# Expert operands of a fused attention and mixture-of-experts kernel, turned by VectorE's 32x32 blocks and by DMAs in place of TensorE

## The chip, the cores and the metric

The kernel runs on one core of a Trainium2 chip. The metric is the device time of one execution in microseconds, and lower is better. Before the change it is 1012.5 us, the median of three runs between 1011.4 and 1016.2.

## The reference

Three stages follow one another, all in float32. The attention lets a query see only the keys of its own bucket:

```python
mask = q_bucket[:, :, :, None] == k_bucket[:, :, None, :]
scores = np.where(mask, scale * np.matmul(q, k.transpose(0, 1, 3, 2)), -1000000000.0)
attn = softmax(scores)                     # batch 2, 8 heads, 768 tokens, head size 64
x = np.matmul(attn, v)                     # laid out as 1536 tokens x 512
```

The expert stage sends each of the 1536 tokens to the best two of 8 experts:

```python
noisy = x @ w_gate + np.log1p(np.exp(x @ w_noise)) * noise
for e in range(8):
    for k in range(2):
        mask = top2[:, k] == e
        h = np.maximum(x[mask] @ w1[e], 0.0)             # 512 -> 1024
        out[mask] += top2_w[mask, k, None] * (h @ w2[e])   # 1024 -> 512
```

The last stage computes `g(x @ w_in) @ w_out` for all tokens, with 2048 columns between and g a quotient of polynomials.

## The kernel before

The whole kernel is one block with a program for each engine, and semaphores between them; the order of work on an engine is the order in which its code is written. The change lies in the expert stage, between attention (to about 320 us) and the last stage (from about 715 us).

**Slots.** Tokens of one expert are gathered in tiles of 128 rows. There are 31 slots of one tile each, in the order of the experts; a table says which expert a slot has. With these inputs the experts 0 to 6 have 4, 3, 4, 3, 4, 4 and 3 slots, and expert 7 has the rest. `slots` unrolls the first and last slots and loops over the others, two at a time.

**One slot.** ScalarE issues the load of the tile's rows, `xg` (L766). TensorE turns them with 4 matmuls on the identity (`turn_x`, L1031) into `ps_m`. VectorE rounds the turned rows to a high part (L1405) and takes the remainder (L1407), both into `xT`. The up product (`up`, L1049) is 24 matmuls, three for each pair of 128 inputs and 512 outputs: high by high, high by remainder of the weights, remainder by high. It fills two banks, `ps_s0`. ScalarE applies relu into `h_sb` (L774), TensorE turns it by 8 matmuls (`turn_h`, L1060) into `ps_s1`, ScalarE rounds (L770) and VectorE takes the remainder (L1411) into `hT`. The down product (`down`, L1074) is 24 matmuls into one bank, `ps_o`; VectorE copies it to `y_sb` (L1417) and ScalarE stores it (L778). On TensorE slot i is: turn h of slot i-1, up product of i, turn x of i+1, down product of i-1.

**Weights.** `w_r` holds two experts in turn, each as a high part and a remainder. A fill (`fill`) belongs to GpSimd: it waits until the last up product of the expert before the previous one is done, issues two casting DMAs of 1 MB for the first half (L529), and splits the first two chunks: a split (L521) subtracts the high part from the raw chunk of 128x1024 and so needs both. Then it waits for that expert's last down product, issues the casts of the second half, and splits the other six chunks. The raw chunks go through a ring of two buffers; SyncE loads them (`stream`, L417), each as soon as the split of the chunk two before is done. After the slots the same code fills `w_out`; its first four splits stand in GpSimd's order behind the gathers of y (L630).

## Time and profile before

| | |
|---|---|
| median of three runs | 1012.5 us |
| profiled execution | 1014.4 us, of which the span is 1012.8 us |
| TensorE busy | 948.4 us, 94% of the span |
| VectorE, ScalarE, GpSimd busy | 593.4, 482.4, 402.4 us |
| moved by DMA | 134.4 MB, 133 GB/s in the mean |

The profile is of one execution. Busy time of an engine is an average over the stages; the chain of waits tells which engine's work sets the end in each of them. A landing is the time from the issue of a DMA until its data is there. The granted clock of TensorE is given as a share of 2.4 GHz.

### The profile page before, as it was taken

The page shows a single profiled execution, that of the slowest core. Times are in us where ns is not written, and L with a number is a line of the kernel's source. Part 1 is how long each engine was busy: PE and PEld are TensorE (multiplying, and loading weights), DVE is VectorE, ACT ScalarE, POOL GpSimd, SP SyncE. Part 2 cuts the span into 40 slices and gives each one's busy share as a digit, 9 for nine tenths or more (in the row PEclk, how much of TensorE's full clock was granted, in tenths as well). Part 3 has the DMA queues.
Part 4 walks back from the last instruction along what each step waited for, and adds up shares of the span by engine and source line. Part 5 has one row for each costly group of instructions (what it writes and reads, how often), then busy time and mean ns, then how long its engine had stood idle before and what let it go on. Part 6 is the DMA issues. An engine that isn't in the chain of part 4 may idle for free.

```text
span 1012.8 us, 17972 instructions
## 1 busy us (share of the span) xinstructions
PE 948.4 (94%) x5797; PEld 815.1 (80%) x5798; DVE 593.4 (59%) x1257; ACT 482.4 (48%) x883; POOL 402.4 (40%) x344
## 2 busy tenths in 40 slices
PE   6999999999891999999999999998489999999998
PEld 4888888888771788888888888887379999999997
DVE  7888888888766222222222222222289878878775
ACT  3677777777660111111111111111177777777775
POOL 4411120111244635544662636610477654463222
PEclk9999999999995999999999999999699999999999
DMA  9752324231133856857775748733621110100000
GB/s 200 220 162 69 84 47 98 52 84 54 63 126 134 282 181 233 286 180 260 266 254 182 248 166 277 282 105 115 194 68 62 33 62 21 53 25 17 32 1 31
DMA packets 102082, 134.42 MB, mean 133 GB/s; under 512 B 55698, under 2 KB 57746, under 8 KB 101522
## 3 DMA queue, kind: packets, MB, share of 16 engines
q1 hardware_dynamic: 73778, 63.01, 20.7%
q0 software_dynamic: 19328, 54.53, 16.4%
q10 hardware_dynamic: 8928, 16.26, 4.7%
q8 instruction: 28, 0.46, 0.2%
q14 instruction: 20, 0.16, 0.1%
HBM read 114.12 MB, written 19.66 MB: 132 GB/s over the span
## 4 chain that ended last, share of the span: by engine, by line
PE 82%; DVE 9%; issue 3%; ACT 2%; POOL 2%; DMA 2%; SPq 0%; DVEq 0%; another core or an unknown queue 0%; ACTq 0%; POOLq 0%
PE ps_s L1049 17%; PE ps_o L1074 17%; PE ps_s L1121 13%; PE ps_t L1107 6%; PE ps_t L919 4%; PE ps_o L932 4%; PE ps_s L1107 3%; PE ps_m L1107 3%; PE ps_s L1060 3%; PE ps_s L910 3%; DVE mx L1201 2%; PE ps_s L911 2%; PE ps_m L885 1%; PE ps_m L1031 1%; PE ps_o L944 1%
## 5 line engine op out<-in xcount | busy, mean ns | idle before, releaser
L521 POOL TENSOR_TENSOR w_r<-raw,w_r 128x1024 f32 (+1 forms) x72 | 171.6, 2399 | 95.9 <-DMA raw<-in_moe_w 41.1
L1049 PE MATMUL ps_s<-w_r,xT 128*128 x744 | 179.1, 397 | 1.8 <-DVE xT L1407 1.8
L1074 PE MATMUL ps_o<-w_r,hT 128*128 x744 | 177.3, 394 | 3.0 <-DVE hT L1411 2.6
L1049 PEld LDWEIGHTS ps_s<-w_r,xT 128*128 128x128 f32 x744 | 139.0, 190 | 29.8 <-issue 2.3
L1074 PEld LDWEIGHTS ps_o<-w_r,hT 128*128 128x128 f32 x744 | 137.5, 188 | 31.0 <-issue 3.5
L1121 PE MATMUL ps_s<-w_r,g_r 128*128 128x512 f32 x576 | 145.4, 397 | 4.5 <-DVE g_r L1491 4.5
L1121 PEld LDWEIGHTS ps_s<-w_r,g_r 128*128 128x128 f32 x576 | 107.6, 190 | 25.1 <-issue 4.3
L770 ACT ACTIVATE hT<-ps_s 128x1024 fp32r<-128x1024 f32 x31 | 31.8, 1027 | 174.3 <-PE ps_s L1060 87.8
L641 POOL TENSOR_TENSOR m<-q,g_r 128x384 f32<-128x384 f32 x64 | 65.9, 1030 | 113.6 <-DVE g_r L1479 113.3
L700 ACT ACTIVATE prob<-ps_s,nb,sc 128x768 f32<-128x768 f32 x96 | 95.3, 993 | 22.5 <-DVE nb L1206 21.8
L774 ACT ACTIVATE h_sb<-ps_s 128x1024 f32<-128x1024 f32 x31 | 31.8, 1027 | 151.8 <-PE ps_s L1049 151.8
L1417 DVE COPY y_sb<-ps_o 128x512 f32<-128x512 f32 x31 | 21.4, 691 | 137.2 <-PE ps_o L1074 137.2
L556 POOL TENSOR_TENSOR qm<-qs,nought 64x384 fp32r<-64x384 f32 x32 | 26.0, 819 | 175.5 <-DVE qs L1176 175.5
L1201 DVE TENSOR_REDUCE mx<-ps_s 128x1 f32<-128x768 f32 x96 | 91.4, 952 | 2.7 <-PE ps_s L911 1.0
L1405 DVE CAST xT<-ps_m 128x512 fp32r<-128x512 f32 x31 | 21.4, 692 | 118.5 <-PE ps_m L1031 118.5
L693 ACT ACTIVATE probT<-ps_t 128x768 f32<-128x768 f32 x93 | 74.9, 806 | 29.3 <-PE ps_t L919 29.3
L919 PE MATMUL ps_t<-ident,prob 128*128 128x128 f32 x570 | 79.6, 276 | 0.3 <-DVE probT L1233 0.3
L910 PE MATMUL ps_s<-km,qm 128*128 128x512 f32 x192 | 73.7, 385 | 0.1
L1107 PE MATMUL ps_t<-x2T,w_r 128*128 (+1 forms) x384 | 72.3, 337 | 0.0
L932 PE MATMUL ps_o<-probT,v_in 128*64 128x128 f32 x1128 | 71.9, 277 | 0.0
L1107 PEld LDWEIGHTS ps_t<-x2T,w_r 128*128 128x128 f32 x384 | 68.2, 188 | 2.6
L1457 DVE SCALAR_TENSOR_TENSOR v<-s,ab,t 128x384 f32<-128x384 f32 x64 | 48.5, 757 | 37.2 <-ACT t L820 37.2
(242 smaller groups left out, 1584.8 us busy)
## 6 DMA issues: line engine op xcount, KB each, us to landing
w_r<-in_moe_w POOLq DMA_DIRECT2D x32, 1024.0 KB, 8.1
raw<-in_moe_w SPq DMA_DIRECT2D x56, 512.0 KB, 3.6
xg<-x_slots ACTq DMA_DIRECT2D x31, 256.0 KB, 3.1
y_slots<-y_sb ACTq DMA_DIRECT2D x31, 256.0 KB, 4.6
q_in<-in_q SPq DMA_DIRECT2D x16, 384.0 KB, 4.0
k_in<-in_k SPq DMA_DIRECT2D x16, 384.0 KB, 5.0
raw<-in_moe_w SPq DMA_DIRECT2D x16, 256.0 KB, 4.3
raw<-in_moe_w_in SPq DMA_DIRECT2D x8, 512.0 KB, 4.9
```

What stands on the lines that cost most here:

```text
L521: pool.tensor_tensor(of_chunk(buf, 1, n), raw[:, par, :], of_chunk(buf, 0, n).bitcast(F), ALU.subtract).then_inc(split_done, 1)
L641: pool.tensor_tensor(m2[:], q2[:, f % 2, :], g_r[:, f % 4, 0, :].bitcast(F), ALU.mult).then_inc(m_ready, 1)
L693: act.activation(probT[:, hh, t % 2, :], src[:, 0:S], ACT.Copy).then_inc(pt_ready[hh], 1)
L700: act.activation(prob[:, hh, t % 2, :], ps_s[hh][:, 0:S], ACT.Exp, bias=nb[:, i:i + 1], scale=sc[:, i:i + 1], accum_out=rs[:, t, hh:hh + 1 ...
L910: pe.matmul(o, qm[:, par, hh, rows], km[:, par, hh, c0:c1], start=True, stop=False)
L919: mm = pe.transpose(to[:, u * P:(u + 1) * P], prob[:, hh, t % 2, u * P:(u + 1) * P], ident[:])
L932: mm = pe.matmul(to[64 * hh:64 * hh + 64, 0:P], v_in[:, par, hh, u * D:(u + 1) * D], probT[:, hh, t % 2, u * P:(u + 1) * P], start=(u == 0 ...
L1049: mm = pe.matmul(ps_s[0][:, o * 512:o * 512 + 512], xT[:, part, c * P:c * P + P], w_r[:, buf, wpart, col:col + 512], start=(c == 0 and par ...
L1074: mm = pe.matmul(ps_o[:, :], hT[:, part, c * P:c * P + P], w_r[:, buf, wpart, col:col + DM], start=(c == 0 and part == 0 and wpart == 0), ...
L1107: mm = pe.matmul(ps_a[f % 4], w_r[:, 0, wpart, c * FF2 + f * P:c * FF2 + f * P + P], x2T[:, par, part, c, :], start=(c == 0 and wpart == 0 ...
L1121: mm = pe.matmul(ps_b[j], g_r[:, f % 4, part, j * P:j * P + P], w_r[:, 1, wpart, f * DM:f * DM + DM], start=(f == 0 and part == 0 and wpar ...
L1201: dve.tensor_reduce(mx[:, i:i + 1], ps_s[hh][:, 0:S], AX.X, ALU.max).then_inc(row_max_done[hh], 1)
```

## The change

TensorE no longer turns anything in the slots. For x, ScalarE loads the rows in four DMAs, one for each group of 32 partitions (a quadrant), which put the 32x32 blocks where a turn inside each quadrant completes the turn of the whole tile; the writes of `x_sb` are laid out so that 32 columns that a quadrant gets stand together. VectorE's 32x32 transpose then makes the turned tile in `ps_m`, and ScalarE instead of VectorE writes the high part.

For h, VectorE turns the blocks as they leave PSUM (`h_t`). Sixteen DMAs of 32 partitions by 1 KB move the blocks between the quadrants into `h_blk`: 12 issued by SyncE, 4 by ScalarE. ScalarE applies relu and rounds (`hT`, high part), and VectorE takes the remainder in four pieces, with relu in the same instruction. `h_t`, `h_blk`, `hT` and `xT` have two buffers, and the up products go to `ps_s0` and `ps_s1` in turn. The down product of a slot comes two slots after its up product, not one.

SyncE is given to the moves, so GpSimd loads the raw chunks itself, after the split that frees the buffer and a small marker instruction.

```diff
-    x_sb = at("x_sb", 144 * KB, [P, NT, DM], F)
+    x_sb = at("x_sb", 144 * KB, [P, NT, Q, DC, P // Q], F)
...
-        body(1, None, 1, False, True)
-        body(2, None, 0, True, True)
-        with eng.Fori(0, (SLOTS - 5) // 2) as g:
-            body(g * 2 + 3, g, 1, True, True)
-            body(g * 2 + 4, g, 0, True, True)
-        for i in range(SLOTS - 2, SLOTS):
-            body(i, (i - 3) // 2, i % 2, True, False)
+        for i in range(4):
+            body(i, i // 2, i % 2)
+        with eng.Fori(0, (SLOTS - 7) // 2) as g:
+            body(g * 2 + 4, g + 2, 0)
+            body(g * 2 + 5, g + 2, 1)
+        for i in range(SLOTS - 3, SLOTS):
+            body(i, i // 2, i % 2)
+
+    def quad_move(g, a, par):
+
+        n = P // Q
+        return (h_blk[g * n:g * n + n, par, a * (FF // Q):(a + 1) * (FF // Q)],
+                h_t[a * n:a * n + n, par, g * (FF // Q):(g + 1) * (FF // Q)])
+
+    def has(i, less):
+
+        return not isinstance(i, int) or i >= less
+
+    def quads(z):
+
+        return z.rearrange("p (a c j) -> p c a j", a=Q, j=P // Q)
+
+    def chunks(z):
+
+        return z.rearrange("p (c a j) -> p c a j", a=Q, j=P // Q)
...
-            def stream(e, chunk):
-                for n in range(CHUNKS):
-                    sp.wait_ge(split_done, e * CHUNKS + n - RING + 1)
-                    load_raw(n % 2, chunk(n))
-
-            with sp.Fori(1, E) as e:
-                stream(e, lambda n: expert_chunk(e, n))
-            stream(E, in_chunk)
-            stream(E + 1, out_chunk)
+            def move_h(i, half, par):
+
+                sp.wait_ge(h_turned, i + 1)
+                for g in range(Q - 1):
+                    for a_ in range(Q):
+                        sp.dma_start(*quad_move(g, a_, par)).then_inc(h_moved[par], 16)
+
+            slots(sp, move_h)
...
+            def load_raw(par, src):
+                dst = raw[:, par, :]
+                if len(src.shape) == 3:
+                    dst = dst.rearrange("p (c d) -> p c d", d=DM)
+                pool.dma_start(dst, src).then_inc(chunk_loaded[par], 16)
+
+            def chunks_of(e):
+                return lambda n: expert_chunk(e, n)
+
+            def split_some(e, buf, some, here, nxt):
+
+                for n in some:
                     if n % 2 == 0:
                         pool.wait_ge(hi_loaded[n // 2], e * 16 + 16)
-                    split(buf, n, n % RING, (e + 1) * (CHUNKS // RING * 16) + n // RING * 16 + 16)
+                    split(buf, n, n % RING, (e - 1) * (CHUNKS // RING * 16) + n // RING * 16 + 16)
+                    if n + RING < CHUNKS or nxt:
+                        pool.wait_ge(split_done, e * CHUNKS + n + 1)
+                        pool.tensor_tensor(mark[:, 3 + n % RING:4 + n % RING], p_col[0:1, :], p_col[0:1, :], ALU.add)
+                        load_raw(n % RING, here(n + RING) if n + RING < CHUNKS else nxt(n + RING - CHUNKS))
...
+            pool.wait_ge(split_done, CHUNKS)
+            for n in range(RING):
+                load_raw(n, expert_chunk(1, n))
...
-                act.dma_start(xg[:, par, :], x_slots[bass.ds(row, P), :]).then_inc(xg_loaded[par], 16)
-
-            def hT_hi_out(i):
+                if has(i, 2):
+                    act.wait_ge(x_turned, i - 1)
+                for g in range(Q):
+                    quad = slice(g * (P // Q), (g + 1) * (P // Q))
+                    act.dma_start(xg[quad, par, :].rearrange("i (a m) -> i a m", a=Q),
+                                  x_slots[bass.ds(row, P), g * P:g * P + P].rearrange("(a i) m -> i a m", a=Q)).then_inc(xg_loaded[par], 16)
+
+            def xT_hi_out(i, par):
+                act.wait_ge(x_turned, i + 1)
+                if has(i, 2):
+                    act.wait_ge(h_ready, i)
+                act.activation(xT[:, par, 0, :], ps_m[:, :], ACT.Copy).then_inc(xT_hi, 1)
+
+            def move_h(i, par):
+
                 act.wait_ge(h_turned, i + 1)
-                act.activation(hT[:, 0, :], ps_s[1][:], ACT.Copy).then_inc(hT_hi, 1)
-
-            def relu(i):
-                act.wait_ge(h_ready, i + 2)
-                act.activation(h_sb[:], ps_s[0][:], ACT.Relu).then_inc(relu_done, 1)
+                if has(i, 2):
+                    act.wait_ge(hT_ready, i - 1)
+                for a_ in range(Q):
+                    act.dma_start(*quad_move(Q - 1, a_, par)).then_inc(h_moved[par], 16)
+
+            def hT_hi_out(i, half, par):
+
+                act.wait_ge(h_moved[par], half * (16 * Q * Q) + 16 * Q * Q)
+                if has(i, 2):
+                    act.wait_ge(slot_done, i)
+                act.activation(chunks(hT[:, par, 0, :]), quads(h_blk[:, par, :]), ACT.Relu).then_inc(hT_hi, 1)
...
-            def act_slot(i, half, par, y, nxt):
-                hT_hi_out(i - 1)
-                relu(i)
-                if not (isinstance(i, int) and i + 2 >= SLOTS):
-                    load_xg(i + 2, par)
-                if y:
+            def act_slot(i, half, par):
+                if not isinstance(i, int) or i + 1 < SLOTS:
+                    xT_hi_out(i + 1, 1 - par)
+                if not isinstance(i, int) or i + 3 < SLOTS:
+                    load_xg(i + 3, 1 - par)
+                if has(i, 1):
+                    hT_hi_out(i - 1, half - (1 - par), 1 - par)
+                move_h(i, par)
+                if has(i, 2):
                     store_y(i - 2, par)
...
-            turn_x(0, 0, 0)
-            up(0)
-            turn_x(1, 0, 1)
-
-            def pe_slot(i, half, par, y, nxt):
-                turn_h(i - 1)
-                up(i)
-                if not isinstance(i, int) or i + 1 < SLOTS:
-                    turn_x(i + 1, half, 1 - par)
-                down(i - 1)
+            def pe_slot(i, half, par):
+                up(i, par)
+                if has(i, 2):
+                    down(i - 2, par)
...
+            def turn_x(i, half, par):
+
+                dve.wait_ge(xg_loaded[par], half * (16 * Q) + 16 * Q)
+                if has(i, 1):
+                    dve.wait_ge(xT_ready, i)
+                dve.transpose(chunks(ps_m[:, :]), quads(xg[:, par, :])).then_inc(x_turned, 1)
+
+            def split_x(i, par):
                 dve.wait_ge(xT_hi, i + 1)
-                dve.tensor_tensor(xT[:, 1, :], ps_m[:, :], xT[:, 0, :].bitcast(F), ALU.subtract).then_inc(xT_ready, 1)
-
-            def split_h(i):
+                dve.tensor_tensor(xT[:, par, 1, :], ps_m[:, :], xT[:, par, 0, :].bitcast(F), ALU.subtract).then_inc(xT_ready, 1)
+
+            def turn_h(i, half, par):
+
+                dve.wait_ge(h_ready, i + 2)
+                if has(i, 2):
+                    dve.wait_ge(h_moved[par], half * (16 * Q * Q))
+                dve.transpose(h_t[:, par, :].rearrange("p (g c i) -> p c g i", g=Q, i=P // Q),
+                              chunks(ps_s[par][:, :])).then_inc(h_turned, 1)
+
+            def split_h(i, par):
                 dve.wait_ge(hT_hi, i + 1)
-                dve.tensor_tensor(hT[:, 1, :], ps_s[1][:], hT[:, 0, :].bitcast(F), ALU.subtract).then_inc(hT_ready, 1)
-
-            def copy_y(i, n, par):
+                for a_ in range(Q):
+                    lo, hi = [hT[:, par, part, :].rearrange("p (c a i) -> p c a i", a=Q, i=P // Q)[:, :, a_, :] for part in (1, 0)]
+                    x = dve.scalar_tensor_tensor(out=lo, in0=h_blk[:, par, a_ * (FF // Q):(a_ + 1) * (FF // Q)].rearrange("p (c i) -> p c i", i=P // Q),
+                                                 scalar=0.0, in1=hi.bitcast(F), op0=ALU.max, op1=ALU.subtract)
+                x.then_inc(hT_ready, 1)
...
-            split_x(0)
-            split_x(1)
-
-            def dve_slot(i, half, par, y, nxt):
-                split_h(i - 1)
+            turn_x(0, 0, 0)
+            split_x(0, 0)
+
+            def dve_slot(i, half, par):
                 if not isinstance(i, int) or i + 1 < SLOTS:
-                    split_x(i + 1)
-                copy_y(i - 1, (i - 1) // 2, 1 - par)
+                    turn_x(i + 1, half + par, 1 - par)
+                    split_x(i + 1, 1 - par)
+                if has(i, 1):
+                    split_h(i - 1, 1 - par)
+                turn_h(i, half, par)
+                if has(i, 2):
+                    copy_y(i - 2, half - 1, par)
```

The loop body of VectorE in the slots, before (one slot of two; `hT` is the turned h, `xT` the turned x):

```order
L1411 TENSOR_TENSOR hT<-ps_s,hT 128x1024
L1404 REGISTER_ALU
L1405 CAST xT<-ps_m 128x512
L1407 TENSOR_TENSOR xT<-ps_m,xT 128x512
L1414 REGISTER_ALU
L1416 ISA
L1417 COPY y_sb<-ps_o 128x512
```

and of the changed kernel (L1438 turns x, L1442 is x's remainder, L1456 h's remainder, L1449 turns h):

```order
L1438 STREAM_TRANSPOSE ps_m<-xg 128x512
L1441 REGISTER_ALU
L1442 TENSOR_TENSOR xT<-ps_m,xT 128x512
L1453 REGISTER_ALU
L1456 SCALAR_TENSOR_TENSOR hT<-h_blk,hT 128x8x32 x4
L1448 REGISTER_ALU
L1449 STREAM_TRANSPOSE h_t<-ps_s 128x8x4x32
L1463 ISA
L1464 COPY y_sb<-ps_o 128x512
```

The remainder of h of the slot before now stands ahead of the turn of h of this slot, and the copy of y behind both.

GpSimd in a fill, from the casts of the second half on, before:

```order
L529 ISA
L529 DMA w_r<-in_moe_w 128x4x512
L529 ISA
L529 DMA w_r<-in_moe_w 128x4x512
L520 REGISTER_ALU
L521 ISA
L521 TENSOR_TENSOR w_r<-raw,w_r 128x1024
L521 ISA
L521 TENSOR_TENSOR w_r<-raw,w_r 128x1024
```

and of the changed kernel:

```order
L542 ISA
L542 DMA w_r<-in_moe_w 128x4x512
L542 ISA
L542 DMA w_r<-in_moe_w 128x4x512
L533 REGISTER_ALU
L534 ISA
L534 TENSOR_TENSOR w_r<-raw,w_r 128x1024
L606 REGISTER_ALU
L607 TENSOR_TENSOR mark<-p_col 1x1
L593 DMA raw<-in_moe_w 128x2x512
L534 ISA
L534 TENSOR_TENSOR w_r<-raw,w_r 128x1024
```

Between two splits there are now a marker and the issue of a DMA.

SyncE's program in the slots is, in the changed kernel, the moves alone (the rows of 12 are the two slots of the loop):

```order
L474 DMA h_blk<-h_t 32x256 x48
L375 UNCONDITIONAL_BRANCH
L375 ISA
L474 DMA h_blk<-h_t 32x256 x12
L471 REGISTER_ALU
L474 DMA h_blk<-h_t 32x256 x12
```

Before, it was the raw chunks of the weights; these are gone from it.

## Rows read from the trace of the kernel before

**Rows 1.** The page: the span.
```profile
span 1012.8 us, 17972 instructions
```

**Rows 2.** Chain that ended last, two slots: start us, us, what, count.
```profile
421.96 0.87 PE ps_s L1060 x8
422.83 5.46 PE ps_s L1049 x24
428.30 0.44 PE ps_m L1031 x4
428.73 5.48 PE ps_o L1074 x24
```

**Rows 3.** The same chain: the first group of matmuls of the slots.
```profile
326.10 7.86 PE ps_s L1049 x24
```

**Rows 4.** The same chain where the slots end and products begin.
```profile
703.31 0.89 PE ps_s L1060 x8
...
706.76 5.72 PE ps_o L1074 x24
...
727.44 7.96 DMA raw<-in_moe_w_out
```

**Rows 5.** Groups by line and shape, 322 to 714 us.
```profile
L1411 DVE TENSOR_TENSOR hT<-ps_s,hT 128x1024 fp32r<-128x1024 f32 x31 | 38.0, 1225 | 34.6 <-ACT hT L770 34.6
...
L770 ACT ACTIVATE hT<-ps_s 128x1024 fp32r<-128x1024 f32 x31 | 31.8, 1027 | 174.3 <-PE ps_s L1060 87.8 <-DVE y_sb L1417 86.4
...
L1407 DVE TENSOR_TENSOR xT<-ps_m,xT 128x512 fp32r<-128x512 f32 x31 | 21.4, 691 | 1.1
```

**Rows 6.** L766, loads of xg, issued by ScalarE.
```profile
DMA to landing us min/median/max: 2.5/3.1/6.9
```

**Rows 7.** L778, stores of y, issued by ScalarE.
```profile
DMA to landing us min/median/max: 2.0/4.6/6.8
```

**Rows 8.** Tile raw, 322 to 714 us: durations in ns min/median/max.
```profile
L417 SPq DMA_DIRECT2D raw<-in_moe_w x54: 332/372/384, 333.0 to 621.9; - x54
```

**Rows 9.** GpSimd's own order, parts of the weight fills: start us, us, work [idle before].
```profile
385.28 0.18 POOL L611 TENSOR_TENSOR mark<-p_col 1x1 f32<-1x1 f32 x1 [5.53 <-PE ps_o L1074]
...
422.04 0.18 POOL L611 TENSOR_TENSOR mark<-p_col 1x1 f32<-1x1 f32 x1 [2.53 <-PE ps_o L1074]
422.63 1.54 POOL L529 DMA_DIRECT2D w_r<-in_moe_w  x2 [0.41 <-issue]
...
441.78 2.39 POOL L521 TENSOR_TENSOR w_r<-raw,w_r 128x1024 f32 x1 [0.24 <-DMA raw<-in_moe_w]
452.88 0.18 POOL L607 TENSOR_TENSOR mark<-p_col 1x1 f32<-1x1 f32 x1 [8.72 <-PE ps_s L1049]
...
460.67 4.76 POOL L521 TENSOR_TENSOR w_r<-raw,w_r 128x1024 f32 x2 [5.64 <-DMA w_r<-in_moe_w]
...
605.84 0.18 POOL L611 TENSOR_TENSOR mark<-p_col 1x1 f32<-1x1 f32 x1 [5.70 <-PE ps_o L1074]
```

**Rows 10.** All engines, 720 to 741 us: VectorE beside GpSimd.
```profile
720.74 0.75 DVE L1438 SCALAR_TENSOR_TENSOR x_first<-y_first,wts,ps_s 128x512 f32<-128x512 f32 x1 [7.55 <-DMA y_first<-y_slots,y_pos_i]
...
734.78 0.62 DVE L1457 SCALAR_TENSOR_TENSOR v<-s,ab,t 128x384 f32<-128x384 f32 x1 [5.03 <-ACT t L820]
...
735.53 4.74 POOL L521 TENSOR_TENSOR w_r<-raw,w_r 128x1024 fp32r<-128x1024 f32 x2 [5.81 <-DMA raw<-in_moe_w_out]
...
737.85 2.83 DVE L1457 SCALAR_TENSOR_TENSOR v<-s,ab,t 128x384 f32<-128x384 f32 x1 [0.16 <-ACT t L820]
```

**Rows 11.** Windows: PE, PEld, DVE, ACT, POOL busy, PEclk, DMA share, GB/s.
```profile
322.00:334.00 12.00, 8.99 (x30) 7.05 (x31) 1.38 (x2) 0.02 (x1) 6.56 (x6) 0.64 0.80 263
364.00:413.00 49.00, 49.00 (x242) 40.93 (x241) 13.20 (x16) 8.21 (x8) 24.01 (x17) 1.00 0.69 234
429.00:434.00 5.00, 5.00 (x23) 4.09 (x22) 1.15 (x2) 0.36 (x1) 0.66 (x1) 1.00 1.12 397
...
703.00:706.70 3.70, 1.18 (x10) 0.85 (x8) 1.91 (x2) 1.02 (x1) 0.00 (x0) 1.00 1.07 332
```

More of the change, by code:

```diff
@@ L32 @@
 DC, FC, FC2 = DM // P, FF // P, FF2 // P
+Q = 4
 WCOLS = DC * FF
@@ L121, in fused_kernel @@
     ab = small("ab", [P, 6], F)
-    mark = small("mark", [1, 3], F)
+    mark = small("mark", [1, 3 + RING], F)
     nought = small("nought", [P, 1], F)
@@ L608, in fill @@
                 cast_hi(buf, *first_half, 0)
-                split_some(e, buf, range(2))
+                split_some(e, buf, range(2), here, nxt)
                 pool.wait_ge(slot_done, start + 1)
@@ L1023, in _, with up @@
             pe.wait_ge(tables_ready, 1)
-            def turn_x(i, loads, par):
-                rows = xg[:, par, :]
-                pe.wait_ge(xg_loaded[par], (i // 2 if isinstance(i, int) else loads + 2) * 16 + 16)
-                if not isinstance(i, int) or i > 0:
-                    pe.wait_ge(xT_ready, i)
-                for c in range(DC):
-                    mm = pe.transpose(ps_m[:, c * P:c * P + P], rows[:, c * P:c * P + P], ident[:])
-                mm.then_inc(x_turned, 1)
             def expert_of(i):
                 return pe.value_load(slot_e[0:1, bass.ds(i, 1)], min_val=0, max_val=E - 1)
-            def up(i):
+            def up(i, par):
                 e = expert_of(i)
@@ L1053, in up, with down @@
                 mm.then_inc(h_ready, 1)
-            def turn_h(i):
-                pe.wait_ge(relu_done, i + 1)
-                if not isinstance(i, int) or i > 0:
-                    pe.wait_ge(hT_ready, i)
-                for c in range(FC):
-                    mm = pe.transpose(ps_s[1][:, c * P:c * P + P], h_sb[:, c * P:c * P + P], ident[:])
-                mm.then_inc(h_turned, 1)
-            def down(i):
+            def down(i, par):
                 e = expert_of(i)
@@ L1414, in copy_y @@
+            def copy_y(i, half, par):
                 dve.wait_ge(slot_done, i + 2)
-                if not isinstance(i, int) or i >= 2:
-                    dve.wait_ge(y_stored[par], n * 16)
+                if has(i, 2):
+                    dve.wait_ge(y_stored[par], half * 16)
                 dve.tensor_copy(y_sb[:, par, :], ps_o[:, :]).then_inc(y_ready, 1)
-            split_x(0)
-            split_x(1)
-            def dve_slot(i, half, par, y, nxt):
-                split_h(i - 1)
+            turn_x(0, 0, 0)
```

84 lines of the change are left out of this document (40 added, 44 removed).

## The prediction

> **What bounds the kernel now.** I read the chain of waits first, since it says whose work a change must shorten. From the first expert matmul at 326.1 us to the last at 706.76 + 5.72 = 712.5 us it is TensorE: in a slot 0.87 us of turning h, 5.46 us of up product, 0.44 us of turning x, 5.48 us of down product, with no gap between them [rows 2 to 4]. That is 12.25 us a slot, and the seven marks that open GpSimd's second half-fill say the same: from the mark of expert 2's fill to that of expert 7's, 605.84 - 385.28 = 220.6 us, are 18 slots [rows 9]. So the stage is TensorE's, 386.4 us of the 1012.8 [rows 1]. The clock there is full [rows 11]. The groups by line give the durations of what runs beside it [rows 5], and the landings and the windows show the other shared thing, the DMA engines: busy 0.69 on average while weights stream, above 1 in a burst of casts [rows 11].
>
> **What TensorE loses.** 12 transposes a slot go, 0.87 + 0.44 = 1.31 us. The order shows nothing but 48 matmuls a slot left. The new stage, if TensorE never waits: first up 7.86 [rows 3] + 30 x 5.46 + 31 x 5.48 = 341.5 us. At the end three down products stand in a row on one bank, so two of them wait for a copy, 0.69 us [rows 5] and a hand-off, 1.6 us together: 343.1. Of the 3.4 us from 703.31 to the last down group [rows 4] nothing else is left. Saved: 386.4 - 343.1 = 43.3 us.
>
> **What h's new way costs.** The turn of h now leaves PSUM by VectorE, crosses partitions in 16 DMAs of 32 KB, 12 from SyncE and 4 from ScalarE, and comes back through ScalarE's relu and VectorE's remainder. VectorE is in order, and the remainder of slot i-1 stands ahead of the turn of slot i. So turn, moves, relu, remainder and the next turn are one closed loop, and no slot can be shorter than its length, two slots of delay in the down product or not. Its length with the DMA engines free:
> - turn, 1024 columns out of PSUM: no row has this operation; the nearest is the 1024-column VectorE pass at 1.23 us [rows 5], the lower end; two passes, 2.46, are the upper. I take 1.23. The Trainium skill, "Vector Engine (DVE) Microarchitecture Reference", on the reshape block, says that the 32x32 transpose sustains one element per cycle and lane, which speaks for the lower end; no row here shows it.
> - moves: SyncE needs 0.33 to 0.38 us for an issue of 512 KB [rows 8], I take 0.37; 11 of them before the last are 4.1 us. The shortest landing of a 256 KB store is 2.0 us, the shortest of a load 2.5 [rows 6, 7]; I take 2.0 (bounds 1.2 and 3). ScalarE's four are issued meanwhile. Sum 6.1.
> - relu, 1.03, as the pass of ScalarE over as many columns [rows 5].
> - remainder: four pieces of 256 columns. 384 columns take 0.62 and 512 take 0.75 [rows 10], 1 ns a column, so 0.49 each, 1.96 in all.
> - hand-offs, 5 x 0.04 us: 0.2.
>
> Sum 10.5 us, against 10.94 for TensorE's two products: 0.4 us to spare. Idle, the loop hides; but it is not idle.
>
> **What lies on the loop when weights stream.** Slots 0 to 25 or so have fills beside them. (a) A fill issues two pairs of 1 MB casts; with expert 1's there are 15 such pairs, each filling the DMA engines for over 5 us, and the moves need 6.1 us of each 11 to 12, so nearly every pair meets one. What a transfer then loses: the landing of y goes from 2.0 (lowest) to 4.6 (median) and 6.8, that of xg from 2.5 to 3.1 and 6.9 [rows 6, 7]. I take y's median, +2.6, as y too queues behind others: 15 x 2.6 = 39 us. Ends: 0.6 (xg's median) and 4.8 (y's highest). (b) The 11 other slots meet single raw chunks: I take 1.0 each, 11 us (ends 0.6 and 2.6). (c) The remainder has now both inputs in SBUF. The one place before where VectorE does that beside a weight split shows 2.83 us instead of 0.62: it sat until GpSimd's pass was over [rows 10]. GpSimd splits 8 x 2.39 = 19 us of a fill of 3.6 slots = 39 us, half the time, and the mean wait is half a pass, 1.2: 0.6 us x 26 = 16 us (ends 0 and 1.2 a slot). Sum 66 us. The two slots of delay swallow part of it once: the turn may be late until its end plus y's copy meets the next down product, 10.94 - 1.23 - 0.69 = 9.0 us; and the spare 0.42 x 26 = 11 us goes off. TensorE waits 66 - 11 - 9 = 46 us.
>
> A rule that speaks against the change: the Trainium skill, "SBUF — State Buffer", section Door 1: The DMA port swizzle, has a transfer of 32 partitions reach 8 of the 16 ports, at 27.2 GB/s each. By it 32 KB take 0.15 us, not 0.08, the 16 moves 1.2 us more where engines are full, and an estimate from it is 15 x 1.2 = 18 us on top, 1037 instead of 1019. No transfer of before is of that shape, and the sum leaves it out.
>
> **The other parts.** The raw chunks now go through GpSimd: the same bytes on the same DMA engines, so no bandwidth is won. Per chunk it adds a mark 0.18, an issue near 0.6 (half of a pair of casts at 1.54 is 0.77, as that is twice the size) and about 0.5 of waits and registers (0.41 before the casts) [rows 9]: 1.3 us. What queues behind it is the next split. A fill costs GpSimd now 444.2 - 422.0 = 22.1 us and 465.4 - 452.9 = 12.5 us, 34.7 in all [rows 9]; 8 x 1.3 adds 10.4, of which about 4 fall into waits for raw data that stand there now: 41 us. Hidden while a fill has over 41 us, 3.6 slots of 11.4 or more; under my forecast of about 12 it is. After the slots it isn't: the chain there runs over the raw chunks of the output weights and the splits behind them (7.96 us of DMA [rows 4]); the issue before chunk 2's landing and two more between splits add 3.3 us. At the start, x is loaded in 4 issues of 0.37 instead of one and turned by VectorE in 0.69 instead of 4 matmuls: +0.6 us. The new layout of x_sb leaves sizes and counts of its writes as they are: nothing, covered by TensorE.
>
> **Sum.** -43.3 + 46 + 3.3 + 0.6 = +6.6 us. The profiled execution took 1014.4 us, its span and 1.6 around it, so 1021.0; it lay 1.9 above the median of 1012.5, on which I forecast: 1019.1 us. About 0.5% is what a measurement of this kernel can tell from no change.
>
> **Rivals.**
> - *The loop hides whole.* If DMA engines serve small transfers between the packets of the casts, moves lose 0.6 us at most per meeting: 15 x 0.6 + 11 x 0.6 - 11 - 9 is below 0, and -39.4 gives 973. For it: xg's median is only 0.6 over its lowest [rows 6]. Against: y's is 2.6 over.
> - *GpSimd's chain takes the end.* With the loop hidden, TensorE leaves 18 x 10.94 / 5 = 39.4 us per fill, GpSimd needs 41: 5 x 1.7 = 8 us less some 2 of initial slack, 979; if it also waits for VectorE's remainders (1.2 us) and for the moves' share of DMA (2 us), 44.5 per fill, it is 998. Also, after a slot product frees the second buffer half, a three-slot expert leaves one slot, 10.94 us, for mark, casts and two splits, 0.2 + 0.4 + 1.5 + 4.8 + 1.3 = 8.2: just enough. Against: a fill now waits idle 8.7 and 5.7 us [rows 9].
> - *Slower by much: moves wait out whole bursts.* If a DMA engine finishes what other queues hold before it takes 12 small transfers, a meeting costs 4.8 us (y's highest) and a raw chunk 2.6: 72 + 29 + 16 - 11 - 9 = 97 us, and 1070. From 2.2 us per meeting on the kernel is slower than before. Waits of 3 us don't lower the clock (granted 1.00 over the gap of 2.6 us before the last group); after the 13 us before the stage it was at its lower level, 0.64 in the mean, and the first group took 7.86 instead of 5.46 [rows 3, 4, 11]. A turn of 2.46 us gives the same size, 1.2 x 26 = 31 us more: 1050.
> - *That the transposes stay.* The order of TensorE has none left in the slots: no chance given.
>
> **Chances.** Forecast (loop paces, 1003 to 1035): 0.55, of which 0.07 faster by over 0.5% (below 1007.4), 0.18 within, 0.30 slower (above 1017.6). Loop hidden 0.15 and GpSimd's chain 0.15: faster. Much slower: 0.15. Together faster 0.37, within 0.18, slower 0.45. The range leaves out half of the hidden case below and two thirds of the much slower one above: 980 to 1048; the likeliest case alone, 1003 to 1035.
>
> **What would show it.** Right: TensorE's idle time in the slots is some 45 us and ends with VectorE's remainder of hT or copy of y; slots with casts beside them last 13 to 15 us, the last five 10.9; ScalarE's hT pass waits for h_blk's DMA; no matmul on the identity in the slots. The issue step is wrong if SyncE's 12 take under 3.5 or over 5 us; the burst step, if moves land as fast beside casts as without; the lock, if the four remainders always take 2 us; GpSimd's, if up products wait for splits. The whole is wrong if every slot takes 10.94 us, or if the last five, with idle DMA engines, take over 11.5.

## The result: 13.9% slower

The changed kernel takes 1156.15 us in the median of four runs (1148.85 to 1158.64), the kernel before 1013.67 beside it: a ratio of 1.139, with a 95% interval of 1.133 to 1.145. The forecast was 1019.1 us, the range 980 to 1048. The profiled execution has a span of 1153.5 us against 1012.8 [rows 1], 140.7 us more. The ratios are of fast runs alone, so that one of the ten runs of raw_gp, which took 2415.2 us where the nine others took 1011.2 to 1016.2, is left out of its ratio.

The page of the changed kernel: busy time of the engines, the span in 40 slices, and the shares of the chain that ended last, by engine and by line.
```profile
span 1153.5 us, 18212 instructions
...
PE 957.7 (83%) x5425; PEld 806.7 (70%) x5426; DVE 683.2 (59%) x1381; ACT 470.3 (41%) x883; POOL 464.9 (40%) x486
...
PE   6999999999465877678676968778547999999998
...
PEclk9999999999777897889897979988777999999999
DMA  9832323302396577757777675863434111010000
...
PE 41%; SPq 17%; DVE 16%; DMA 11%; issue 7%; ACT 4%; POOL 2%; DVEq 1%; ACTq 0%; POOLq 0%
SPq L474 17%; PE ps_s L1150 11%; DMA h_blk<-h_t 10%; PE ps_t L1136 5%; DVE hT L1456 5%; PE ps_t L971 4%; PE ps_o L984 3%; DVE h_t L1449 3%; ACT hT L823 3%; PE ps_s L1136 3%; PE ps_m L1136 3%; DVE mx L1230 2%; PE ps_s L962 2%; PE ps_o L1109 2%; PE ps_s L963 2%
```
TensorE's row has a hollow from the 12th slice to the 30th, the expert slots (323.8 to 849.9 us), and the chain no longer runs through the slots' matmuls but through SyncE's queue (SPq, 17%), the landing of h's moves (10%) and VectorE. Where the chain stood on TensorE without a gap [rows 2], this is one turn of the loop now (start us, us, what; 504 to 519 us; seven more issues of 0.6 us and short pieces are left out at the dots):
```profile
504.38 1.17 DVE h_t L1449
...
505.57 0.51 SPq L474
...
506.12 0.59 SPq L474
...
511.20 0.59 SPq L474
...
511.84 0.59 SPq L474
...
512.47 1.84 DMA h_blk<-h_t
...
514.41 1.07 ACT hT L823
...
516.51 0.42 DVE hT L1456
516.93 1.17 DVE h_t L1449
```
Turn, eleven issues and a twelfth with its landing, relu, remainder, next turn: 12.54 us, in a slot with nothing in its way. The same by instruction (durations in ns min/median/max, first and last start), then VectorE's row at 528 us, where GpSimd's split 527.72 to 530.14 stands beside the four pieces of the remainder, and the waits from 340 to 850 us (us in total, times, longest):
```profile
L474 SPq DMA_DIRECT2D h_blk<-h_t x372: 507/592/1956, 332.9 to 837.3; - x186
...
L1456 DVE SCALAR_TENSOR_TENSOR hT<-h_blk,hT x124: 409/419/3374, 347.9 to 841.2; 128x256 fp32r<-128x256 f32 x124
...
L1449 DVE STREAM_TRANSPOSE h_t<-ps_s x31: 1234/1236/1250, 331.7 to 828.8; 128x1024 f32<-128x1024 f32 x31
```
```profile
515.50 1.43 DVE L1456 SCALAR_TENSOR_TENSOR hT<-h_blk,hT 128x256 fp32r<-128x256 f32 x4 [5.14 <-ACT hT L823]
...
528.11 3.32 DVE L1456 SCALAR_TENSOR_TENSOR hT<-h_blk,hT 128x256 fp32r<-128x256 f32 x4 [4.88 <-ACT hT L823]
```
```profile
ACT hT L823 <- DMA h_blk<-h_t: 219.3, 30, 15.3
...
PE ps_o L1109 <- DVE y_sb L1464: 121.1, 26, 10.6
POOL mark L640 <- PE ps_o L1109: 118.2, 7, 23.0
```
The 31 turns of h give the period: (828.8 - 331.7) / 30 = 16.57 us, where the 31 remainders of before came every 12.27. Read off VectorE's and ScalarE's rows slot by slot, its mean is made up of turn 1.24, from the turn's end to the relu 11.13 (least 8.76, most 16.09), relu 1.09, from there to the next turn 3.11 (least 1.34, most 6.46). GpSimd waits 118 us for slots, so it isn't late here. TensorE's granted clock was 0.86 in the mean over 330 to 850 us, but the chain passes TensorE there hardly at all.

### The profile page after: what moved, and what is told of

The parts are those of the page before. It is cut to its first block, busy times and chain, and to the rows that moved or that the text cites. A ratio compares the mean times of both kernels' runs of the same rounds, so it can differ in the third digit from the quotient of the medians.

```text
span 1153.5 us, 18212 instructions
## 1 busy us (share of the span) xinstructions
PE 957.7 (83%) x5425; PEld 806.7 (70%) x5426; DVE 683.2 (59%) x1381; ACT 470.3 (41%) x883; POOL 464.9 (40%) x486
## 4 chain that ended last, share of the span: by engine, by line
PE 41%; SPq 17%; DVE 16%; DMA 11%; issue 7%; ACT 4%; POOL 2%; DVEq 1%; ACTq 0%; POOLq 0%
SPq L474 17%; PE ps_s L1150 11%; DMA h_blk<-h_t 10%; PE ps_t L1136 5%; DVE hT L1456 5%; PE ps_t L971 4%; PE ps_o L984 3%; DVE h_t L1449 3%; ACT hT L823 3%; PE ps_s L1136 3%; PE ps_m L1136 3%; DVE mx L1230 2%; PE ps_s L962 2%; PE ps_o L1109 2%; PE ps_s L963 2%
## 5 line engine op out<-in xcount | busy, mean ns | idle before, releaser
L1109 PE MATMUL ps_o<-w_r,hT 128*128 x744 | 222.2, 465 | 132.8 <-DVE y_sb L1464 121.1
L1109 PEld LDWEIGHTS ps_o<-w_r,hT 128*128 128x128 f32 x744 | 170.3, 232 | 184.4 <-issue 144.8
L1456 DVE SCALAR_TENSOR_TENSOR hT<-h_blk,hT 128x256 fp32r<-128x256 f32 x124 | 96.9, 842 | 230.4 <-ACT hT L823 230.4
L1092 PE MATMUL ps_s<-w_r,xT 128*128 x744 | 175.9, 393 | 17.1 <-DVE xT L1442 17.0
L823 ACT ACTIVATE hT<-h_blk 128x1024 fp32r<-128x1024 f32 x31 | 32.8, 1059 | 223.9 <-DMA h_blk<-h_t 219.3
L808 ACT ACTIVATE xT<-ps_m 128x512 fp32r<-128x512 f32 x31 | 18.6, 599 | 252.2 <-issue 240.8
L1442 DVE TENSOR_TENSOR xT<-ps_m,xT 128x512 fp32r<-128x512 f32 x31 | 21.4, 692 | 93.5 <-ACT xT L808 93.5
L984 PEld LDWEIGHTS ps_o<-probT,v_in 128*64 128x64 f32 x1128 | 60.6, 137 | 9.3 <-issue 8.2
```

Of the source, the lines that this page charges most:

```text
L984: mm = pe.matmul(to[64 * hh:64 * hh + 64, 0:P], v_in[:, par, hh, u * D:(u + 1) * D], probT[:, hh, t % 2, u * P:(u + 1) * P], start=(u == 0 ...
L1092: mm = pe.matmul(ps_s[par][:, o * 512:o * 512 + 512], xT[:, par, part, c * P:c * P + P], w_r[:, buf, wpart, col:col + 512], start=(c == 0 ...
L1109: mm = pe.matmul(ps_o[:, :], hT[:, par, part, c * P:c * P + P], w_r[:, buf, wpart, col:col + DM], start=(c == 0 and part == 0 and wpart == 0),
L1456: x = dve.scalar_tensor_tensor(out=lo, in0=h_blk[:, par, a_ * (FF // Q):(a_ + 1) * (FF // Q)].rearrange("p (c i) -> p c i", i=P // Q), sca ...
```

## Experiments

The period is that of VectorE's turn of h, or of its remainder of h in kernels without one. A row without an interval is a single run. The runs of the kernel before beside them had medians of 1011.8 to 1018.0 us.

| run | us | ratio, 95% interval | period us |
|---|---|---|---|
| changed kernel | 1156.2 | 1.133 to 1.145 | 16.57 |
| nolock | 1112.2 | | 15.20 |
| small | 1134.6 | | 15.85 |
| quiet | 1127.2 | | 15.64 |
| few | 1028.3 | | 12.29 |
| late | 1036.7 | 1.017 to 1.026 | 12.64 |
| late_raw | 1041.0 | | 12.59 |
| late_quiet | 1023.7 | | 12.01 |
| late_few | 1024.5 | | 12.00 |
| late_psum | 1024.5 | 1.007 to 1.014 | 12.22 |
| psum_quiet | 992.6 | | 10.92 |
| bounce | 1046.4 | 1.025 to 1.037 | 12.97 |
| bounce_quiet | 1046.3 | | 12.86 |
| bounce_psum | 1072.1 | 1.051 to 1.064 | 13.87 |
| bounce_last | 1045.0 | 1.025 to 1.033 | 12.52 |
| raw_gp | 1014.7 | 1.001 to 1.004 | 12.25 |
| x_only | 997.8 | 0.984 to 0.988 | 11.82 |

### Is it the number of issues, the bytes, or the loop itself?

**few.** In SyncE's loop (ScalarE's part likewise):
```
-                    for a_ in range(Q):
-                        sp.dma_start(*quad_move(g, a_, par)).then_inc(h_moved[par], 16)
+                    cols = slice(g * (FF // Q), (g + 1) * (FF // Q))
+                    sp.dma_start(h_blk[:, par, cols], h_t[:, par, cols]).then_inc(h_moved[par], 16)
```


> The sixteen quadrant moves of a slot are four DMAs of 128 partitions by 256 columns (three by SyncE, one by ScalarE): the same bytes, a quarter of the issues. The crossing of the quadrants is left out, so h stays turned by blocks only. Issue count as the price (0.63 us each in a row): free loop falls from 12.4 to some 7 us, below TensorE's 11, turns of h every 11 to 13 us, 1000 to 1050 us. Bytes or collisions with the weights' transfers as the price: the moves take as long as now, 8.8 us free and 11.1 on average, and the time stays above 1120 us.

**small.**
```
-        return (h_blk[g * n:g * n + n, par, a * (FF // Q):(a + 1) * (FF // Q)],
-                h_t[a * n:a * n + n, par, g * (FF // Q):(g + 1) * (FF // Q)])
+        m = FF // Q // 8
+        return (h_blk[g * n:g * n + n, par, a * (FF // Q):a * (FF // Q) + m],
+                h_t[a * n:a * n + n, par, g * (FF // Q):g * (FF // Q) + m])
```


> Sixteen quadrant moves as now, but each brings 32 of its 256 columns (a block's other columns stay zero, so most of h is left out). Issue count as the price: each of SyncE's twelve still takes 0.55 to 0.63 us, the shortest period stays near 12 us, and the time falls by no more than what of the 2.4 us per slot of collisions goes, to 1080 to 1150 us. Bytes as the price: moves take under 5 us, turns of h every 11 to 13 us, 1000 to 1050 us.

Both came out as expected for the count of issues. The same bytes in a quarter of the issues take 128 us off; an eighth of the bytes in the same issues takes 22 off. SyncE's issues of h's moves, in few (128 KB each) and in small (4 KB each):
```profile
L474 SPq DMA_DIRECT2D h_blk<-h_t x93: 464/602/1217, 333.1 to 702.9; - x93
```
```profile
L475 SPq DMA_DIRECT2D h_blk<-h_t x372: 507/591/1445, 335.2 to 817.8; - x186
```
One issue is 0.59 to 0.60 us whether it moves 4, 32 or 128 KB. The shortest period of small is 12.43 us, as in the changed kernel (12.44); that of few is 7.57. So the loop is priced by the count of issues. What the bytes of the moves themselves add, in collisions with other transfers, is 0.7 us of the period (16.57 against 15.85).

**late.** VectorE's row (in ScalarE's the high part goes last too):
```
-                if has(i, 1):
-                    split_h(i - 1, 1 - par)
                 turn_h(i, half, par)
                 if has(i, 2):
                     copy_y(i - 2, half - 1, par)
+                if has(i, 1):
+                    split_h(i - 1, 1 - par)
```


> Order alone: VectorE does the turn of h of a slot and the copy of y before the remainder of the slot before, and ScalarE issues its moves and the store before that slot's high part, so that a block of h has two slots' time to land. Nothing else differs from the changed kernel. Closed loop (turn 1.24, twelve issues of 0.63 us one behind another on SyncE with the landing behind them, 8.8 free and 11.1 on average, high part 1.1, remainder 1.3 to 3.5, then the next turn): the loop opens, what remains per slot is the larger of TensorE's 11 us and SyncE's 7.6 us of issues, so turns of h come every 11 to 12.5 us in place of 16.57, and the time falls by 31 x 4 to 5.5 us, to 980 to 1030 us. If bytes on the DMA engines, the shared port with GpSimd, GpSimd's own chain or the lower clock set the 16.57 us, the order changes little of it: over 1110 us.

No instruction is taken away, and 119 us go, 84% of the loss. So it was the loop and not the amount of work, bytes or clock. The time is 7 us above what I expected, and the period 12.64 is still not TensorE's; that is the question of the third part.

### The other terms of the loop

**nolock.**
```
-                    x = dve.scalar_tensor_tensor(out=lo, in0=h_blk[:, par, a_ * (FF // Q):(a_ + 1) * (FF // Q)]...
+                    x = dve.scalar_tensor_tensor(out=lo, in0=ps_t[:, (a_ % 2) * (FF // Q):(a_ % 2 + 1) * (FF // Q)]...
```


> The remainder of h takes its first operand from a PSUM bank in place of h's block in SBUF, so that the instruction has one input in SBUF (its values are then not h's: that part of the computation is left out). If what holds it beside GpSimd's splits is the pair of SBUF inputs, the four pieces take 1.3 to 1.5 us always, turns of h come every 14.8 us in place of 16.57, and the time falls by 1.8 x 31 = 55 us, to 1090 to 1110 us. If that waiting were the main cause of the loss, to below 1050 us. If two inputs aren't what is held, no change: 1150 us.

```profile
L1456 DVE SCALAR_TENSOR_TENSOR hT<-ps_t,hT x124: 411/414/426, 347.2 to 799.2; 128x256 fp32r<-128x256 f32 x124
```
Not one of 124 pieces is held, where before the longest took 3.37 us. From relu to the next turn it is always 1.33 us, in place of 3.11 on average; the moves took 0.4 us more, so the period fell by 1.4 and not 1.8, and the time came out 2 us above the range. The Trainium skill, "SBUF — State Buffer", section SBUF: two separate sides, calls VectorE's and GpSimd's shared port pair an exclusive lock, which a VectorE instruction with two inputs in SBUF takes against a GpSimd one that reads SBUF. The trace agrees: the same instruction with one input in SBUF is never held.

**quiet.** The fills' casts: `src[:, part * c:part * c + c, :g // less]` with less = 8.

> The changed kernel, but the casts of the weights of the experts from the third on and of the next stage bring an eighth of their columns (most of those weights are left out). If the moves' excess of 2.4 us over their 8.8 us free is collisions with the casts: period 14.2 us in place of 16.57, less 31 x 2.4 = 74 us, 1075 to 1100 us. If the bytes of the weights were the cause of the whole loss: below 1040 us. If the excess has another cause (raw chunks, GpSimd's hold on the SBUF port): above 1120 us.

The remainder of each weight takes up what its cast leaves, so that little of the sum is left out. A miss: 29 us, where I expected 56 to 81. From turn to relu the mean goes from 11.13 to 10.58, so the casts' bytes are a quarter of the 2.4 us of collisions; the other 0.4 us by which the period fell are shorter waits of the remainder. The collisions aren't only the casts' doing: x's loads, y's stores and raw chunks stand in the same queues, and no run here parts them.

### What holds the opened loop at 12.6 us?

A fill of GpSimd waits for a slot of TensorE's twice, before the casts of each half: seven fills, fourteen such gates. In late GpSimd waits at one of them only, and fills follow one another as fast as it can do them: the marks that open them stand at 369.45 and, six later, 668.54, 49.9 us each. TensorE stops in late in two ways (from 360 to 701 us, stops of over 0.3 us): ten down products start 0.3 us after a remainder of h that took 3.4 to 6.2 us, 16.5 us of stops, and up products wait four times for GpSimd's splits, 20.0 us. Three runs tried to shorten that or to rule out SyncE.

**late_quiet** (late, with quiet's casts), **late_raw** (late, raw chunks of an eighth of the columns), **late_few** (late, with few's moves).

> The run late with the casts of the weights from the third expert on bringing an eighth of their columns (the remainder takes up what they leave, coarser). In the run late GpSimd never waits for its slot gates and a fill follows the other every 49.9 us (369.45 to 668.54 us, six fills), so that GpSimd's chain sets the time. If so, the casts' landings (38.7 us of its waits) and some of the raw chunks' (54.5 us) go, fills come every 38 to 43 us, slots at TensorE's 11 to 11.5 us: 985 to 1010 us. If the opened loop is held by VectorE, SyncE or the clock: 1030 to 1040 us.

> The run late with the raw chunks bringing an eighth of their columns (most of the remainders of the weights are then wrong: that part is left out); GpSimd issues as many loads as before. If the raw chunks' bytes and their landings lengthen GpSimd's chain (54.5 us of waits), fills come every 40 to 44 us: 990 to 1015 us. If GpSimd's own instructions (remainder 2.4, mark and issue 1.3 us, eight times, and the casts' issues and landings, 43 to 46 us a fill) are the chain, 1015 to 1030 us. If neither, 1035 us.

> The run late with four moves of 128 partitions in place of sixteen (same bytes; the crossing of the quadrants is left out). With the loop opened, SyncE's 7.6 us of issues fit in a slot, so their number should no longer count: 1025 to 1040 us, fills every 47 to 50 us as in the runs few and late. If SyncE's issues still hold the slots: 990 to 1015 us.

late_quiet lies between its two ranges, late_few 0.5 us below the first of its two, and late_raw 6 us above the 1035 us for "neither". Without the raw chunks' bytes GpSimd's wait for them falls from 54.5 to 21.5 us, but the period stays, 12.59: no up product waits for a split any more, and in exchange the stops behind the held remainder grow from 16.5 to 35.8 us (from 360 to 701 us), since splits that don't wait for their chunks stand closer together (a remainder took up to 6.7 us). With four moves the period is 12.00, with small casts 12.01, and the remainder is held in both. None of them alone is the bound.

**bounce.** h crosses through DRAM, five issues by ScalarE for sixteen, and SyncE streams the raw chunks again:
```
+                act.dma_start(h_pages[par], h_t[:, par, :]).then_inc(h_stored[par], 16)
...
+                for g in range(Q):
+                    act.dma_start(h_blk[g * (P // Q):(g + 1) * (P // Q), par, :].rearrange("i (a m) -> i a m", a=Q),
+                                  h_pages[par, :, g * (FF // Q):(g + 1) * (FF // Q)].rearrange("(a i) m -> i a m", a=Q))
```


> Both expert operands turned by VectorE as in the changed kernel, in the order of the run late, but h crosses the quadrants through DRAM: ScalarE issues one store of h's turned block and, a slot later, four loads in place of sixteen moves; SyncE brings the raw chunks again and GpSimd issues none. If the run late is held by GpSimd's chain (50 us a fill with its own raw issues, marks and landings, in the stretch 574 to 625 us) and the issues are the price of the moves: the slots run at TensorE's two products, 11.0 to 11.8 us, and the time falls below that of the kernel before, to 975 to 1005 us. If the extra bytes (1 MB a slot through DRAM where the moves carry 0.5 MB) collide with the weights, fills come late and the time is 1010 to 1050 us.

> The run bounce with the casts of the weights from the third expert on bringing an eighth of their columns. If the DMA engines' load (busy share 0.9 and more in the stage, raw chunks landing in 5.3 us where they took 4.4 in the run late) is what holds that kernel, the time falls to 985 to 1010 us. If ScalarE's row (nine issues and three instructions a slot) holds it: 1035 to 1048 us.

Both came out at 1046, in the second range of each. But the cause that I had given for that range of bounce_quiet, ScalarE's row, isn't what its trace shows. TensorE's row, then VectorE's, from 574 to 599 us:
```profile
577.28 5.60 PE L1108 MATMUL ps_o<-w_r,hT 128*128 x24
582.72 5.60 PE L1091 MATMUL ps_s<-w_r,xT 128*128 x24
591.42 7.33 PE L1108 MATMUL ps_o<-w_r,hT 128*128 x24 [3.10 <-issue]
```
```profile
574.64 1.43 DVE L1455 SCALAR_TENSOR_TENSOR hT<-h_blk,hT 128x256 fp32r<-128x256 f32 x4 [1.81 <-ACT hT L819]
...
585.43 5.70 DVE L1455 SCALAR_TENSOR_TENSOR hT<-h_blk,hT 128x256 fp32r<-128x256 f32 x4 [1.81 <-ACT hT L819]
```
While GpSimd doesn't split, a slot is 10.97 us. Beside two splits (585.09 to 589.83) the remainder takes 5.70 us in place of 1.43, and the down product that needs it starts 3.10 late, then runs its 24 matmuls in 7.33 instead of 5.60 us: the granted clock is 1.00 from 577 to 591.4 us, the wait included, and 0.77 from 591.4 to 598.8. So it is in the whole stage: up to 700 us 19 of TensorE's 20 stops of over 0.3 us end 0.3 us after a remainder of h, and 18 of these remainders took 2.9 to 5.8 us in place of 1.43.

**late_psum.** ScalarE writes the relu into the free two banks of PSUM, and the remainder is one instruction with one input in SBUF:
```
+                act.activation(chunks(ps_t[:, :]), quads(h_blk[:, par, :]), ACT.Relu).then_inc(h_relued, 1)
...
+                act.activation(hT[:, par, 0, :], ps_t[:, :], ACT.Copy).then_inc(hT_hi, 1)
...
+                dve.tensor_tensor(hT[:, par, 1, :], ps_t[:, :], hT[:, par, 0, :].bitcast(F), ALU.subtract)
```


> The run late, with the remainder of h read from PSUM: ScalarE writes relu of the crossed block into the free two banks, then the high part from there, and VectorE subtracts in one instruction with one input in SBUF (1.23 us in the kernel before) in place of four with two. In the run bounce_quiet the slots without a split beside them took 10.97 us (two products of 5.44) and a slot in which the four pieces took 5.70 in place of 1.43 us, beside two of GpSimd's splits, stopped TensorE 3.10 us. If that hold is what keeps the opened loop at 12.6 us: 11.2 to 11.8 us a slot as far as GpSimd's fills (49.9 us each) allow, 1005 to 1030 us. If GpSimd's chain alone is the bound: 1030 to 1040 us.

**psum_quiet** (late_psum with quiet's casts).

> The run late_psum with the casts from the third expert on bringing an eighth of their columns. In late_psum GpSimd waits at none of its gates after the first and a fill follows the other every 47.1 us; with the casts cut, in the run late_quiet, every 44.0 us with waits at five gates. If GpSimd's chain and the held remainder together are what the opened loop loses, slots come at 10.9 to 11.3 us between fills: 990 to 1005 us. If something else holds the slots: 1015 to 1025 us, as either cure alone gave.

Both times fell into the ranges expected. late_psum falls by 12 us, to where GpSimd's chain holds it (marks at 372.62 and 654.95: 47.1 us a fill, no gate waited for after the first; up products wait 29.5 us for splits). The remainder took 1.22 to 1.23 us in all 31 slots. With that relieved too, the chain of psum_quiet is TensorE's alone, slot after slot:
```profile
504.16 5.44 PE ps_s L1097 x24
509.60 5.46 PE ps_o L1114 x24
515.06 5.44 PE ps_s L1097 x24
520.50 5.53 PE ps_o L1114 x24
```
Its period, 10.92 us, is the 10.94 of two products. So the opened loop lost its time to two things at once, the held remainder and GpSimd's chain of fills, which is why one cure alone gave 12 us, the other 13, and both together 44 (late_quiet and psum_quiet are single runs).

**bounce_psum, bounce_last.** bounce with the remainder from PSUM; in bounce_psum the high part also stands ahead of the stores in ScalarE's row.

> The run bounce with the same remainder from PSUM, and the high part ahead of the two stores in ScalarE's row. GpSimd's chain isn't lengthened here and TensorE waited for nothing but the held remainder in the slots looked at: slots of 11.0 to 11.6 us, 975 to 995 us, below the run x_only. If the 1 MB a slot through DRAM (DMA busy share over 0.9) delays the raw chunks enough to set the time: 1010 to 1045 us.

> The run bounce_psum with the high part of h as the last thing in ScalarE's row of a slot, as in the run bounce. In bounce_psum ScalarE waited for h's loads a few us after it issued them (160.9 us of waits, 29 times), since store, loads, relu and high part stood in one slot: a closed loop again, through ScalarE. If that alone made it 1072: the slots go back under bounce's 13.0 us, and without the held remainder to 11 to 12 us: 985 to 1015 us. If the load on the DMA engines (busy share 0.9) holds it: 1025 to 1046 us.

bounce_psum missed both of its ranges, bounce_last fell into the second, that for full DMA engines. In bounce_psum I closed a loop again: turn, ScalarE's store, its loads, the relu and the high part, which now had to come before ScalarE's next store:
```profile
ACT ps_t L822 <- DMA h_blk<-h_pages: 160.9, 29, 14.3
```
bounce_last undoes that and gains 27 us, but stays at 1045. Its row for 350 to 700 us (PE, PEld, DVE, ACT, POOL, granted clock, DMA share, GB/s) has full DMA engines, where late_psum, which loads as many bytes of weights, has 0.89 and 259 GB/s:
```profile
350.00:700.00 350.00, 317.10 (x1323) 255.41 (x1323) 121.48 (x139) 72.92 (x83) 164.75 (x102) 0.96 1.00 298
```
Two things come late in it: the raw chunks, for which GpSimd waits 82.5 us (46.3 in late_psum), and h's blocks, for which ScalarE waits 122.7 us up to 720 us; down products stop behind a remainder that took 1.23 us and so was held by nothing. So h's way through DRAM cost more here than the issues that it saved. That its bytes do it, and not ScalarE's nine issues a slot, is not shown: no run lightens the DMA engines' load in bounce_last.

### The parts of the change that don't touch h

**raw_gp.** The kernel before, with `pool.dma_start(dst, src)` for SyncE's stream of raw chunks.

> The kernel before with only the raw chunks' loads moved from SyncE to GpSimd. By the prediction's terms a fill grows from 34.7 to 41 us and stays hidden, with 3.3 us of tail: 1010 to 1020 us. If a fill grows to the 50 us that the run late shows, it outlasts the three to four slots of 12.25 us of an expert at some turns: 1020 to 1045 us.

**x_only.** The kernel before, with
```
+                dve.transpose(chunks(ps_m[:, :]), quads(xg[:, par, :])).then_inc(x_turned, 1)
```
for the four transposes of x, and the four quadrant loads.

> The kernel before with x alone turned by VectorE (four quadrant loads of x by ScalarE, one turn of 0.7 us); h stays with TensorE, and the raw chunks with SyncE. TensorE loses four of its twelve transposes a slot, 0.44 us, and nothing is added to a loop: 31 x 0.44 = 13.6 us less, 995 to 1005 us. If VectorE's longer row (0.7 us more per slot, 5.5 in 12) or ScalarE's four issues delay the high part or the remainder of h: 1010 to 1025 us.

Both came out as expected. raw_gp costs 0.1 to 0.4%; its tail after the start of the last down matmul is 302.5 us against 300.7. But its fills are 44.3 us apart (marks at 363.90 and 629.62) and five of seven second gates find GpSimd late: it only just fits under 3.6 slots of 12.25 us, 44.1 us, and late shows that it doesn't under shorter ones. x_only gains what was worked out for it, 14.0 us for 13.6, and beats both kernels. TensorE's chain in it:
```profile
423.04 5.44 PE ps_o L1079 x24
428.49 0.87 PE ps_s L1065 x8
429.36 5.46 PE ps_s L1054 x24
434.81 5.45 PE ps_o L1079 x24
```
The slot is the one of [rows 2] without its 0.44 us.

## Why the prediction was wrong

From the rows: the first up product starts at 323.8 in place of 326.10 (-2.3 us), the last down matmul starts at 849.5 in place of 712.1, and from there to the end it is 304.0 us in place of 300.7 (+3.3). So the slots themselves took 139.7 us more:

| term, over 30 periods | predicted us | measured us |
|---|---|---|
| TensorE's transposes gone | -43 with the ends | (12.27 - 10.94) x 30 = -40 |
| free loop above 10.94 | 0, 10.5 is below it | (12.44 - 10.94) x 30 = +45 |
| moves beside other transfers | 50 | (11.13 - 8.76) x 30 = +71 |
| remainder held by GpSimd | 16 | (3.11 - 1.35) x 30 = +53 |
| spare and slack taken off | -20 | 0 |
| the ends of the slots | in the first row | +10.7 |

- **The step that failed is the issue term of the moves.** I took 0.37 us for an issue of SyncE from loads of 512 KB out of DRAM [rows 8]; a move from SBUF to SBUF takes 0.59 and 0.04 to the next, eleven of them are 6.9 us in place of 4.1. The landing was right (1.84 and 0.1 for 2.0), the turn too (1.24 for 1.23), and the remainder was over-priced (1.35 for 1.96). Together 12.44 in place of 10.5 us, and my own test, twelve issues in over 5 us, names it: 7.5. few and small show that it is the count. Of the some 136 us by which the change of the time was above the forecast, this step makes 65 (45 and the 20 taken off), the lock 37, the collisions 21 and the ends 11, by the table above.
- **What made it dear is the sign of a difference.** At 10.5 the loop had 0.4 us to spare under TensorE's 10.94, so that collisions would first use up spare and slack, and only slots with casts would count. At 12.44 every slot is late, and every later microsecond on the loop counts whole: the 20 us taken off weren't there. The forecast rested on two numbers 4% apart, and the shorter one had no row for an issue of this kind; an upper bound beside the 0.37 was missing altogether, though the sum had eleven of them.
- **Collisions** were forecast at 1.9 us a slot and measured at 2.4: the mechanism right, the size near. But quiet says that the casts I priced them by are a quarter of it.
- **The lock** is the second mis-sized term: 1.76 us a slot for 0.6. 20 of 30 slots show it. I took a wait of half a split for half of the slots; but the four pieces are four instructions, each of which can meet a split, and in bounce_quiet two splits in a row held them for 5.70 us. nolock and late_psum show that it is the second input in SBUF.
- **The ends** weren't in the sum: from the last turn of h to the last matmul (moves, relu, remainder, down product) are 20.7 us, where the kernel before had 6.8 from its last remainder; at the first slot the change gained 3.2.
- **Right:** TensorE's saving (x_only, psum_quiet), no wait of an up product for a split, and TensorE waiting for VectorE's copy of y and remainder, though for 121 and 11.5 us and not 46 together. The tail's 3.3 us agree in part by luck: raw_gp, with that part of the change alone, shows 1.8, and the same code after the slots took from 302.8 us (nolock) to 304.5 (psum_quiet). The start was forecast 0.6 us later and came 2.3 earlier; that says nothing of the change, since it lies anywhere from 323.05 (raw_gp, which leaves x as it was) to 327.49 (psum_quiet).
- **The last five turns**, which were to come every 10.9 us and to show the whole wrong if they took over 11.5, came 12.44 to 17.88 us apart. The DMA engines weren't idle there, as I had thought (share 0.50 over 745 to 830 us).
- **The clock.** I wrote that waits of 3 us don't lower it, from one wait of 2.6 us. In bounce_quiet a wait of 3.10 us was followed by 7.4 us at 0.77 in the mean; in the changed kernel the mean was 0.86 over the slots. So a stop of TensorE there cost more than its own length: 3.10 us and another 1.73.
- **Of the rivals** "moves wait out bursts" had the sign and the wrong cause; its 1070 fell short. "GpSimd's chain takes the end" couldn't show while the loop was slower; late and late_psum show it real, at 47 to 50 us a fill in place of the 41 that I worked out from one fill, some of whose waits I thought the added work would fill.

## What to carry to other kernels

Draw the loop that an in-order engine closes over a transfer before summing what it saves: if turn, issue, landing and return stand between two turns of one engine's row, the loop's length is the slot, and a reordering by one slot was worth 119 us here, 8 times what x's part of the change, the one that gained, gave. In such a loop count the DMA issues and price each by a row of the same kind of transfer; where no row has it, the bound must be multiplied by the count before it goes into the range. When the length of a loop is forecast within 5% of the bound beside it, give both signs: below it costs nothing, above it every term counts in full.

## What the runs showed of the hardware

- An issue from SBUF to SBUF took SyncE 0.59 us for 4 KB, 32 KB and 128 KB alike, and ScalarE 0.62 (0.52 to 1.89), against 0.37 for 512 KB from DRAM [rows 8]. ScalarE's store of 512 KB from SBUF to DRAM took 0.36 (bounce_psum) or 0.44 us (bounce) in the median. The Trainium skill, "DMA: Bandwidth & Descriptors", section Anatomy of one DMA — SWDGE (gpsimd) path, puts the sequencer's dispatch at about 50 ns and most of a DMA's fixed 2 us into the receipt of its write; that was written of GpSimd's DMAs, and on SyncE here the issue was a third as long as the landing (0.59 and 1.84 us).
- VectorE's 32x32 turn took 1.24 us for 1024 columns from PSUM to SBUF and 0.70 to 0.72 for 512 from SBUF to PSUM, as long as a remainder over as many columns (1.23 and 0.69 us [rows 5]).
- A VectorE instruction with both inputs in SBUF went from 0.42 to as much as 3.37 us beside GpSimd's splits; with one input from PSUM it was never above 0.43 (nolock).
- After a wait of 3.10 us of TensorE, in which the granted clock was 1.00, it was 0.77 in the mean over the next 7.4 us (bounce_quiet, from 591.4 us).
- A move of 4 KB landed only 0.1 us before one of 32 KB (1.62 us in small and 1.74 in the changed kernel, the shortest of each), so at this size the bytes hardly show. Whether the 32 partitions of a move cost anything where the engines are full, no run here parts from the rest.
